# Second buffer for the sums of w2's pieces, a use-ordered list of their parts, and the fourth token sum split by VectorE in its PSUM bank

## The chip, the cores and the metric

The kernel runs on one core of a Trainium2 chip. The metric is the device time of one execution in microseconds, the median of several runs.

## The reference

Attention over 2 batches, 8 heads, 768 positions and head width 64, with a mask of 8 global and 96 local keys, feeds a mixture of four experts and then a gated block. What matters here is the expert part, computed for 1536 tokens with D = 512 and F = 1024, and the gated part behind it:

```python
for e in range(E):
    h = np.maximum(x @ w1[e], 0.0)
    out += p[:, e:e + 1] * (h @ w2[e])
...
a = x @ w1
b = x @ w2
h = a * b @ w3
return (h @ w_out).astype(np.float32)
```

## The kernel before, in words

**Precision and tiling.** Every fp32 operand is split into a high and a low part (`ah`, `al` for weights, `bh`, `bl` for tokens, `sh`, `sl` for hidden values). One product of two blocks is three matmuls of 128 x 128 by 128 x 384: high by high, low by high, high by low (lines 50 to 52). The high part is made by ScalarE, the low part by GpSimd or VectorE as "raw minus high".

**Seven products instead of eight.** The matrices are taken as 2 x 2 blocks, and a Strassen-Winograd scheme computes the four results c11, c12, c21, c22 from seven products. Weights enter as A11, A12, A22 and sums S1, S2, S3, S4; tokens as B11, B21, B22 and sums T1 to T4. Product 1 is A11 x B11, 2 is A12 x B21, 3 is S4 x B22, 4 is A22 x T4, 5 is S1 x T1, 6 is S2 x T2, 7 is S3 x T3. VectorE joins them: u2 from product 6, u3 from product 7, c22 from 5, c21 from 4, c12 from 3.

**Two halves.** The 1536 tokens are worked in two halves of 768. The first half of the dense part runs until about 477 us. The second half, t = 1, runs the four experts with `second_expert` and then `gated(1)`; the change touches only these.

**One second-half expert.** TensorE first works four groups i0 to i0+3 with w1 (seven products of two k-steps each; a group needs one set of split weights, loaded by SyncE with `load_split` from DRAM, in three ring slots). After each group ScalarE and VectorE rectify c11, c21, c22, which are B11, B21, B22 of the next matrix, and form the sums T1 to T4 of the rectified results (`rectified_sum`): T1 and T2 into `b_sum`, T3 and T4 into `raw[2]`. ScalarE takes the high part of each (`sum_high`), GpSimd the low part (`sum_low`). Then come two groups of w2, j and j+1, with seven products of four k-steps each, k being the group that the tokens come from (`down_group`).

**w2's pieces.** w2 comes in four pieces n0 to n0+3 per expert (two k-steps each), loaded raw into `raw[0]` and `raw[1]` in turn (`load_piece`), because `raw[2]` serves T3 and T4. GpSimd forms S1 to S4 of a piece in four operations (`down_sums`; S1, S2, S4 in `a_sum`, S3 in the piece itself). The piece is split in four parts, numbered by `PARTS`: 0 is A11, A12; 1 is S1, S2; 2 is A22, S3; 3 is S4. ScalarE makes the high part (`down_high`, line 1191), GpSimd the low part (`down_low`, line 1197), in order of piece and then of part. `a_sum` is one buffer, so the sums of a piece wait for the low parts of the one before.

**Order.** Every engine runs one queue written out by hand, in order, and they meet only through counting semaphores. `second_expert_gpsimd`, `second_expert_scalar`, `kept_sums` and `second_expert` are these queues for an expert. `snap` copies product 1 from its bank into `s1`, two buffers by parity of the group. Later `keep_h11` puts the rectified c11 there. `down_snap` does what `snap` does, for w2's groups. SyncE's queue is `sync`: a load whose wait is not met holds all loads behind it.

Of the kernel before, what the change touches and what calls it, by code (L numbers as in the profile page):

```python
# [28 lines left out]
E = 4  # L29
# [788 lines left out]
DOWN_ORDER = (1, 6, 2, 7, 5, 4, 3)  # L818
DOWN_SUMS = ("u2", "u3", "c22", "c21", "c12")
# [3 lines left out]
class Dense:  # L823
# [24 lines left out]
    def __init__(self, nc, sem, lay, bank, weights, folded, gates_dram, x_dram, x_stored, out, fold, g_stored):  # L848
# [55 lines left out]
        self.t_made, self.t_high, self.t_low = sem("t_made"), sem("t_high"), sem("t_low")  # L904
# [47 lines left out]
    def wait_split(self, eng, m):  # L952
        kind, n = self.pieces()[m]
        if kind == "up":
            eng.wait_ge(self.a_raw_low, n + 1)
        elif kind == "down":
            eng.wait_ge(self.dn_low, len(PARTS) * n + 3)
        else:
            eng.wait_ge(self.w2_low, self.w2_count(kind, n) + 1)
# [78 lines left out]
    def sync(self, sp):  # L1038
# [115 lines left out]

    def down_sums(self, pool, n):

        nc, c = self.nc, 4 * n
        raw, s = self.raw_of("down", n), self.a_sum
# [3 lines left out]
        if n:  # L1162
            pool.wait_ge(self.dn_low, len(PARTS) * n)
# [9 lines left out]
    def down_part(self, n, p):  # L1173
# [5 lines left out]
        return self.a_sum[:, to.start - S1 * QUART:to.stop - S1 * QUART], to  # L1179
# [13 lines left out]
    def down_low(self, pool, n, p):  # L1193
        src, to = self.down_part(n, p)
        s = self.slot_down(n)
        pool.wait_ge(self.dn_high, len(PARTS) * n + p + 1)
# [91 lines left out]
    def portion_t2(self, dve, k):  # L1288
        at = slice(k * TT, (k + 1) * TT)
        dve.wait_ge(self.b_summed, 12 + 4 * k + 1)  # L1290
        dve.wait_ge(self.t_low, 4 * KH * E)
# [53 lines left out]
    def bank_free(self, pe, i, c):  # L1345

        if i % UPS < 4 * E and i >= UPS:
            pe.wait_ge(self.t_made, self.t_count(i, {12: T1, 22: T2, 11: T3, 21: T4}[c]))
# [85 lines left out]

    def down_group(self, pe, j, p, ks=range(KH)):
# [12 lines left out]
        for k in ks:  # L1448
            i, n = UPS + KH * e + k, 2 * j + k // 2
            s = self.slot_down(n)  # L1450
            pe.wait_ge(self.dn_low, len(PARTS) * n + [a in part for part in PARTS].index(True) + 1)
            if b >= T1:
                pe.wait_ge(self.t_low, self.t_count(i, b))
# [8 lines left out]
    def second_expert(self, pe, e):  # L1462
# [82 lines left out]
    def gated(self, pe, t):  # L1545
# [77 lines left out]
    def snap(self, act, i):  # L1623
# [3 lines left out]
        elif i >= UPS + 2 and i < UPS + KH * E:  # L1627
            act.wait_ge(self.t_made, self.t_count(i - 2, T1))
# [50 lines left out]
    def t_raw(self, b):  # L1679
        return {T1: self.b_sum[:, 0:TT], T2: self.b_sum[:, TT:2 * TT], T3: self.raw[2][:, 0:TT],  # L1680
                T4: self.raw[2][:, TT:2 * TT]}[b]

    def sum_high(self, act, i, b):
        act.wait_ge(self.t_made, self.t_count(i, b))
        self.nc.scalar.activation(self.sh[b][i % KH][:, :], self.t_raw(b), ACT.Copy).then_inc(self.t_high, 1)  # L1685

    def down_snap(self, act, j):
        e, d = divmod(j, DOWNS)
        act.wait_ge(self.dn_product, self.dn_count(j, 1))
        act.wait_ge(self.t_made, self.t_count(UPS + KH * e + 2 + d, T1))  # L1690
        self.nc.scalar.activation(self.s1[d][:, :], self.bank[3 * d][:, 0:TT], ACT.Copy).then_inc(self.dn_snapped, 1)

    def second_expert_scalar(self, act, e):
        i0, n0 = UPS + KH * e, 4 * e
        for g in range(KH):
# [3 lines left out]
            if g:  # L1699
# [3 lines left out]
                if g >= 2:  # L1703
                    self.down_high(act, n0 + g - 2, 0)
# [17 lines left out]
        for n in (n0 + 2, n0 + 3):  # L1722
            for p in range(len(PARTS)):
                self.down_high(act, n, p)
        self.down_snap(act, DOWNS * e + 1)

    def second_gated_scalar(self, act):
# [151 lines left out]
    def sum_low(self, pool, i, b):  # L1879
        k = i % KH  # L1880
        pool.wait_ge(self.t_high, self.t_count(i, b))
        if b == T4 and k:
            for s in range(2):
                pool.wait_ge(self.y_stored[s], 16 * (ROWS_OUT // 2))
        self.nc.gpsimd.tensor_tensor(self.sl[b][k][:, :], self.t_raw(b), self.sh[b][k][:, :].bitcast(F32),  # L1885
                                     ALU.subtract).then_inc(self.t_low, 1)

    def sums_low(self, pool, i):
        for b in (T1, T2, T3, T4):
# [676 lines left out]
```

## Time and profile before

| | us |
|---|---|
| median of 3 runs (850.46 to 852.68) | 850.75 |
| the profiled execution, its own time | 854.38 |
| its span, first to last instruction | 852.8 |
| TensorE matmuls busy | 805.7 |
| GpSimd busy | 513.2 |
| VectorE busy | 451.9 |
| ScalarE busy | 334.1 |

The mean clock granted to TensorE was 0.981 of full speed. The engines overlap, so the busy times do not add up to the span. In the rows, PE is TensorE, DVE is VectorE, ACT is ScalarE, POOL is GpSimd and SP is SyncE; L1197 is line 1197 of the kernel. A row of a timeline gives the start, the duration, the engine, the line, the operation, output and inputs, and, in brackets, how long the engine idled before and what ended that.

### The profile page before, as it was taken

To read this page: it belongs to the slowest core of one execution; us is meant where nothing else is said; L and a number is where in the kernel's file an instruction comes from. 1 tells how busy PE (TensorE), PEld (TensorE's weight loads), DVE (VectorE), ACT (ScalarE), POOL (GpSimd) and SP (SyncE) were. 2 spreads that over 40 slices of the span, in tenths; PEclk is the share of its full clock that TensorE was granted. 3 is DMA by queue.
4 is the path that set the end of the run, shared out by engine and by line. 5 is a ranking of instruction groups with operands and counts; after the bars stand their busy time and mean duration, and the time that the engine had idled before them with its cause. 6 is when DMAs were issued, how large, how long until landed. Compare 5 with 4: busy or idle time off the path is not lost.

```text
span 852.8 us, 13816 instructions
## 1 busy us (share of the span) xinstructions
PE 805.7 (94%) x4702; PEld 756.8 (89%) x4702; DVE 451.9 (53%) x1002; ACT 334.1 (39%) x706; POOL 513.2 (60%) x476
## 2 busy tenths in 40 slices
PE   9999989999999999999999988996998898899997
PEld 7667758999999999998998988996997898888986
DVE  6776675514425425438664472475485375476620
ACT  4477873513314314323433362163063154322211
POOL 3478995784684675684965189189269449712200
PEclk9999999999999999999999998999999899899999
DMA  8924456773482473561996314634542552556501
GB/s 309 336 101 158 154 201 235 309 282 120 170 324 88 178 296 116 180 267 44 351 375 242 90 66 139 216 109 134 191 138 78 170 193 75 161 195 230 181 14 65
DMA packets 49563, 155.18 MB, mean 182 GB/s; under 512 B 5952, under 2 KB 7248, under 8 KB 49488
## 3 DMA queue, kind: packets, MB, share of 16 engines
q1 hardware_dynamic: 45104, 145.67, 47.5%
q10 hardware_dynamic: 4320, 8.52, 2.9%
q8 instruction: 43, 0.70, 0.3%
q0 software_dynamic: 64, 0.03, 0.1%
q14 instruction: 32, 0.26, 0.1%
HBM read 103.31 MB, written 50.88 MB: 181 GB/s over the span
## 4 chain that ended last, share of the span: by engine, by line
PE 69%; POOL 19%; DVE 5%; issue 3%; ACT 2%; DMA 1%; DVEq 0%; SPq 0%; ACTq 0%; POOLq 0%
PE bank L50 22%; PE bank L52 22%; PE bank L51 22%; POOL al L1197 6%; POOL sl L1885 5%; POOL pr L490 2%; PE bank L602 1%; PE bank L619 1%; PE bank L592 1%; POOL bl L1254 1%; POOL a_sum L1166 1%; POOL raw L1168 1%; POOL a_sum L1171 1%; POOL a_sum L1169 1%; DMA fold_mt_raw<-m3t 1%
## 5 line engine op out<-in xcount | busy, mean ns | idle before, releaser
L50 PE MATMUL bank<-bh,ah 128*128 128x384 f32 x672 | 226.3, 337 | 5.4 <-issue 1.8
L52 PE MATMUL bank<-bh,al 128*128 128x384 f32 x672 | 225.7, 336 | 0.0
L51 PE MATMUL bank<-bl,ah 128*128 128x384 f32 x672 | 225.5, 336 | 0.0
L50 PEld LDWEIGHTS bank<-bh,ah 128*128 128x128 f32 x672 | 126.8, 189 | 7.9 <-DVE hl L2227 2.4
L51 PEld LDWEIGHTS bank<-bl,ah 128*128 128x128 f32 x672 | 126.7, 189 | 0.1
L52 PEld LDWEIGHTS bank<-bh,al 128*128 128x128 f32 x672 | 126.6, 188 | 0.0
L1208 POOL TENSOR_TENSOR w2l<-raw,w2h 128x1024 fp32r<-128x1024 f32 x24 | 57.8, 2414 | 96.1 <-ACT w2h L1203 95.8
L50 PE MATMUL bank<-sh,ah 128*128 128x384 f32 x224 | 80.5, 359 | 26.1 <-POOL al L1197 22.8
L52 PE MATMUL bank<-hh,w2l 128*128 128x384 f32 x256 | 85.6, 335 | 0.0
L51 PE MATMUL bank<-hl,w2h 128*128 128x384 f32 x256 | 85.6, 335 | 0.0
L50 PE MATMUL bank<-hh,w2h 128*128 128x384 f32 x256 | 85.6, 334 | 0.0
L1150 POOL TENSOR_TENSOR al<-raw,ah 128x512 fp32r<-128x512 f32 x48 | 61.0, 1290 | 37.8 <-ACT ah L1130 37.5
L51 PE MATMUL bank<-sl,ah 128*128 128x384 f32 x224 | 79.2, 353 | 0.0
L52 PE MATMUL bank<-sh,al 128*128 128x384 f32 x224 | 78.9, 352 | 0.0
L1885 POOL TENSOR_TENSOR sl<-b_sum,sh 128x384 fp32r<-128x384 f32 x32 | 31.7, 1011 | 75.7 <-ACT sh L1685 75.7
L1634 ACT ACTIVATE parts<-bank 128x384 f32<-128x384 f32 x48 | 23.4, 488 | 124.2 <-PE bank L52 124.2
L50 PEld LDWEIGHTS bank<-sh,ah 128*128 128x128 f32 x224 | 45.2, 202 | 29.9 <-POOL al L1197 25.4
L490 POOL TENSOR_TENSOR pr<-pr,rden 128x512 f32<-128x512 f32 (+1 forms) x48 | 45.5, 972 | 9.0 <-DVE rden L558 9.0
L1998 DVE SCALAR_TENSOR_TENSOR hl<-bank,hh 128x384 fp32r<-128x384 f32 x64 | 35.3, 551 | 26.6 <-ACT hh L1643 26.2
L2019 DVE TENSOR_TENSOR bank<-bank,gate 128x384 f32<-128x384 f32 x24 | 13.4, 560 | 65.9 <-PE bank L52 65.9
L50 PEld LDWEIGHTS bank<-hh,w2h 128*128 128x128 f32 x256 | 48.1, 188 | 0.0
L51 PEld LDWEIGHTS bank<-hl,w2h 128*128 128x128 f32 x256 | 48.1, 188 | 0.0
(157 smaller groups left out, 1679.4 us busy)
## 6 DMA issues: line engine op xcount, KB each, us to landing
raw<-weights SPq DMA_DIRECT2D x56, 512.0 KB, 3.5
splits<-ah SPq DMA_DIRECT2D x24, 896.0 KB, 4.1
splits<-al SPq DMA_DIRECT2D x24, 896.0 KB, 6.4
ah<-splits SPq DMA_DIRECT2D x48, 256.0 KB, 3.4
al<-splits SPq DMA_DIRECT2D x48, 256.0 KB, 4.2
ah<-splits SPq DMA_DIRECT2D x24, 384.0 KB, 4.9
al<-splits SPq DMA_DIRECT2D x24, 384.0 KB, 6.2
k<-k SPq DMA_DIRECT2D x8, 704.0 KB, 6.5
```

Of the source, the lines that this page charges most:

```text
L50: nc.tensor.matmul(out, wh, xh, start=start, stop=False, skip_group_check=adds_on)
L51: nc.tensor.matmul(out, wh, xl, start=False, stop=False, skip_group_check=adds_on)
L52: return nc.tensor.matmul(out, wl, xh, start=False, stop=stop, skip_group_check=adds_on)
L490: self.nc.gpsimd.tensor_tensor(probs, probs, scale, ALU.mult).then_inc(self.normed, 1)
L592: last = self.nc.tensor.matmul(self.scores_of(u, h), self.q[s][head, i * P:(i + 1) * P], self.k[s][head, key0:key0 + self.width(u)], start ...
L1150: last = nc.gpsimd.tensor_tensor(self.al[s][:, c], self.raw_of("up", g)[:, c], self.ah[s][:, c].bitcast(F32), ALU.subtract)
L1197: self.nc.gpsimd.tensor_tensor(self.al[s][:, to], src, self.ah[s][:, to].bitcast(F32), ALU.subtract).then_inc(self.dn_low, 1)
L1208: self.nc.gpsimd.tensor_tensor(self.w2l[:, c], self.raw_of(kind, n)[:, :], self.w2h[:, c].bitcast(F32), ALU.subtract).then_inc(self.w2_low, 1)
L1634: self.nc.scalar.activation(self.s1[i % 2][:, :], self.bank[self.banks(i)[0]][:, 0:TT], ACT.Copy).then_inc(self.snapped, 1)
L1885: self.nc.gpsimd.tensor_tensor(self.sl[b][k][:, :], self.t_raw(b), self.sh[b][k][:, :].bitcast(F32), ALU.subtract).then_inc(self.t_low, 1)
L1998: self.nc.vector.scalar_tensor_tensor(self.hidden(self.hl, i, c), self.c_of(i, c), 0.0, self.hidden(self.hh, i, c).bitcast(F32), ALU.max, ...
L2019: nc.vector.tensor_tensor(bank, bank, gate, ALU.mult).then_inc(self.dn_scaled, 1)
```

## The change

- `down_sums` writes the sums of odd pieces to `raw[2]` and those of even pieces to `a_sum` (`sums_of`), so that a piece waits for the one two before it. GpSimd forms the sums of the next expert's first two pieces behind the current expert.
- The parts of an expert's four pieces are split in the order `DOWN_PARTS`, which runs over pairs of (piece, part), interleaved otherwise than before with the T sums in the queues of ScalarE and GpSimd.
- T3 goes to `s1[i % 2]`, and T4 is written over c21 in its PSUM bank. VectorE makes T4's low part (`t4_split_low`), and a semaphore of its own counts it. GpSimd is left with T1, T2, T3; in the last group T2 comes ahead of T1.
- `snap` and `down_snap` wait for GpSimd's low part of T3 of the group that had this `s1` before.
- TensorE's product orders change in w2's first group j and at the start of the second `gated`.
- SyncE asks for the splits of groups 4 and 5 of the last stage before the piece of w_out that stood between them.

```diff
+DOWN_PARTS = ((0, 0), (0, 2), (0, 1), (0, 3), (1, 0), (1, 1), (1, 2), (1, 3), (2, 0), (2, 1), (3, 0), (3, 1), (2, 2),
+              (3, 2), (2, 3), (3, 3))
...
-        self.load_splits(sp, i0 + 3)
+        for f in range(3, 6):
+            self.load_splits(sp, i0 + f)
         self.load_piece(sp, m + 2)
-        self.load_splits(sp, i0 + 4)
+        self.load_splits(sp, i0 + 6)
         self.load_piece(sp, m + 3)
-        for f in range(5, KF):
-            self.load_splits(sp, i0 + f)
+        self.load_splits(sp, i0 + 7)
...
+    def sums_of(self, n):
+        return self.raw[2][:, 0:3 * QUART] if n % 2 else self.a_sum[:, :]
...
-        if n:
-            pool.wait_ge(self.dn_low, len(PARTS) * n)
+        if n >= 2:
+            pool.wait_ge(self.dn_low, max(self.part_count(n - 2, 1), self.part_count(n - 2, 3)))
...
         self.down_group(pe, j, 5, (0, 1))
-        self.down_group(pe, j, 2, (0, 1))
+        self.down_group(pe, j, 2, (0, 1, 2))
         self.down_group(pe, j, 6, (3,))
-        self.down_group(pe, j, 2, (2, 3))
+        self.down_group(pe, j, 2, (3,))
+        self.down_group(pe, j, 5, (2,))
         self.down_group(pe, j, 7)
-        self.down_group(pe, j, 5, (2, 3))
+        self.down_group(pe, j, 5, (3,))
         self.down_group(pe, j, 4)
...
+            self.product1(pe, i0 + 1)
             self.product5(pe, i0, (0,))
             self.product6(pe, i0, (0,))
             self.product2(pe, i0)
-            self.product1(pe, i0 + 1)
             self.product2(pe, i0 + 1)
             self.product5(pe, i0, (1,))
             self.product6(pe, i0, (1,))
-            self.product5(pe, i0 + 1)
+            self.product5(pe, i0 + 1, (0,))
             self.product7(pe, i0)
-            self.product6(pe, i0 + 1)
+            self.product5(pe, i0 + 1, (1,))
             self.product4(pe, i0)
             self.product3(pe, i0)
+            self.product6(pe, i0 + 1)
...
         elif i >= UPS + 2 and i < UPS + KH * E:
-            act.wait_ge(self.t_made, self.t_count(i - 2, T1))
+            act.wait_ge(self.t_low, self.low_count(i - 2, T3))
...
-    def t_raw(self, b):
-        return {T1: self.b_sum[:, 0:TT], T2: self.b_sum[:, TT:2 * TT], T3: self.raw[2][:, 0:TT],
-                T4: self.raw[2][:, TT:2 * TT]}[b]
+    def t_raw(self, i, b):
+        return {T1: self.b_sum[:, 0:TT], T2: self.b_sum[:, TT:2 * TT], T3: self.s1[i % 2][:, :], T4: self.c_of(i, 21)}[b]
...
-            act.wait_ge(self.t_made, self.t_count(UPS + KH * e + 2 + d, T1))
+            act.wait_ge(self.t_low, self.low_count(UPS + KH * e + 2 + d, T3))
...
+        order = DOWN_PARTS[0:2], DOWN_PARTS[2:4], DOWN_PARTS[4:5], DOWN_PARTS[5:8]
...
-                    self.down_high(act, n0 + g - 2, 0)
+                    for m, p in order[2 * g - 4]:
+                        self.down_high(act, n0 + m, p)
...
-                for p in range(1, len(PARTS)):
-                    self.down_high(act, n0 + g - 2, p)
+                for m, p in order[2 * g - 3]:
+                    self.down_high(act, n0 + m, p)
...
-                self.out_high(act, "last", 4 + f - 2 - f // 4)
+                self.out_high(act, "last", 2 + f - f // 4)
...
     def second_expert_gpsimd(self, pool, e):
...
+        self.sums_low(pool, i0, T1, T2, T3)
+        self.parts_low(pool, e, 0, 2)
+        self.sums_low(pool, i0 + 1, T1, T2, T3)
+        self.parts_low(pool, e, 2, 5)
+        self.sums_low(pool, i0 + 2, T1, T2)
+        self.parts_low(pool, e, 5, 6)
+        self.down_sums(pool, n0 + 2)
+        self.sums_low(pool, i0 + 2, T3)
+        self.parts_low(pool, e, 6, 7)
+        self.sums_low(pool, i0 + 3, T2, T1, T3)
+        self.parts_low(pool, e, 7, 11)
+        self.down_sums(pool, n0 + 3)
+        self.parts_low(pool, e, 11, 16)
         if e < E - 1:
             self.down_sums(pool, n0 + 4)
+            self.down_sums(pool, n0 + 5)
...
+    def t4_split_low(self, dve, i):
+        k = i % KH
+        dve.wait_ge(self.t_high, self.t_count(i, T4))
...
+        self.nc.vector.tensor_tensor(self.sl[T4][k][:, :], self.t_raw(i, T4), self.sh[T4][k][:, :].bitcast(F32),
+                                     ALU.subtract).then_inc(self.t4_low, 1)
...
         self.add_u3_c22(dve, i)
+        if i % KH:
+            self.t4_split_low(dve, i - 1)
         self.add_c21(dve, i)
```

## Rows read from the trace of the kernel before

**Rows 1.** The page, busy time and share of the span of each engine
```profile
PE 805.7 (94%) x4702; PEld 756.8 (89%) x4702; DVE 451.9 (53%) x1002; ACT 334.1 (39%) x706; POOL 513.2 (60%) x476
```

**Rows 2.** TensorE's waits from 480 to 853 us: total us, times, longest
```profile
PE bank L50 <- POOL al L1197: 22.8, 8, 3.6
PE bank L50 <- POOL sl L1885: 3.2, 3, 1.1
```

**Rows 3.** TensorE's timeline of the last second-half expert
```profile
707.51 0.33 PE L50 MATMUL bank<-sh,ah 128*128 128x384 f32 x1
...
712.54 0.34 PE L52 MATMUL bank<-sh,al 128*128 128x384 f32 x1
715.13 0.44 PE L50 MATMUL bank<-sh,ah 128*128 128x384 f32 x1 [2.26 <-POOL al L1197]
...
719.08 0.42 PE L50 MATMUL bank<-sh,ah 128*128 128x384 f32 x1 [1.05 <-POOL sl L1885]
...
732.78 0.69 PE L50 MATMUL bank<-sh,ah 128*128 128x384 f32 x1 [3.55 <-POOL al L1197]
733.27 0.52 PE L51 MATMUL bank<-sl,ah 128*128 128x384 f32 x1
...
748.88 0.34 PE L50 MATMUL bank<-bh,ah 128*128 128x384 f32 x1
```

**Rows 4.** GpSimd's timeline from 487 to 753 us
```profile
487.24 1.99 POOL L1885 TENSOR_TENSOR sl<-b_sum,sh 128x384 fp32r<-128x384 f32 x2 [16.82 <-ACT sh L1685]
...
554.73 1.99 POOL L1885 TENSOR_TENSOR sl<-b_sum,sh 128x384 fp32r<-128x384 f32 x2 [19.25 <-ACT sh L1685]
...
622.31 2.00 POOL L1885 TENSOR_TENSOR sl<-b_sum,sh 128x384 fp32r<-128x384 f32 x2 [19.31 <-ACT sh L1685]
...
690.84 2.00 POOL L1885 TENSOR_TENSOR sl<-b_sum,sh 128x384 fp32r<-128x384 f32 x2 [20.30 <-ACT sh L1685]
...
697.30 1.29 POOL L1197 TENSOR_TENSOR al<-raw,ah 128x512 fp32r<-128x512 f32 x1 [2.21 <-ACT ah L1191]
698.56 1.99 POOL L1885 TENSOR_TENSOR sl<-b_sum,sh 128x384 fp32r<-128x384 f32 x2
...
715.03 1.28 POOL L1197 TENSOR_TENSOR al<-raw,ah 128x512 fp32r<-128x512 f32 x1
716.28 0.73 POOL L1197 TENSOR_TENSOR al<-a_sum,ah 128x256 fp32r<-128x256 f32 x1
...
720.83 0.73 POOL L1166 TENSOR_TENSOR a_sum<-raw 128x256 f32<-128x256 f32 x1
...
723.84 1.31 POOL L1197 TENSOR_TENSOR al<-raw,ah 128x512 fp32r<-128x512 f32 x1
...
752.38 1.41 POOL L1279 TENSOR_TENSOR bl<-x,bh 128x384 fp32r<-128x384 f32 x1 [1.18 <-ACT bh L1274]
```

**Rows 5.** ScalarE's timeline, the fourth group's snap and the first of w2
```profile
701.96 0.47 ACT L1634 ACTIVATE parts<-bank 128x384 f32<-128x384 f32 x1
...
712.57 0.50 ACT L1691 ACTIVATE parts<-bank 128x384 f32<-128x384 f32 x1
```

**Rows 6.** VectorE's timeline, u3 of the fourth group and a split from SBUF
```profile
707.71 0.56 DVE L1964 TENSOR_TENSOR parts<-bank,parts 128x384 f32<-128x384 f32 x1
...
752.92 1.27 DVE L1279 TENSOR_TENSOR bl<-b_sum,bh 128x384 fp32r<-128x384 f32 x1
```

**Rows 7.** SyncE's issues in the last stage; DMA issues from 550 to 760 us (last row)
```profile
774.15 0.32 SPq L968 DMA_DIRECT2D raw<-folded  x1
774.51 0.43 SPq L1030 DMA_DIRECT2D ah<-splits  x1
...
raw<-weights SPq DMA_DIRECT2D x10, 512.0 KB, 3.5
```

**Rows 8.** TensorE's timeline of the last stage, two of its four waits
```profile
762.87 0.44 PE L50 MATMUL bank<-bh,ah 128*128 128x384 f32 x1 [1.39 <-DVE hl L2227]
...
781.12 0.41 PE L50 MATMUL bank<-bh,ah 128*128 128x384 f32 x1 [1.83 <-issue]
```

More of the change, by code:

```diff
@@ L956, in wait_split @@
         elif kind == "down":
-            eng.wait_ge(self.dn_low, len(PARTS) * n + 3)
+            eng.wait_ge(self.dn_low, self.part_count(n, 2))
         else:
@@ L1153, in up_half_low, with part_count @@
             last.then_inc(self.a_raw_low, 1)
+    @staticmethod
+    def part_count(n, p):
+        e, j = divmod(n, 2 * DOWNS)
+        return len(DOWN_PARTS) * e + DOWN_PARTS.index((j, p)) + 1
+    def sums_of(self, n):
+        return self.raw[2][:, 0:3 * QUART] if n % 2 else self.a_sum[:, :]
     def down_sums(self, pool, n):
         nc, c = self.nc, 4 * n
-        raw, s = self.raw_of("down", n), self.a_sum
+        raw, s = self.raw_of("down", n), self.sums_of(n)
         a11, a12, a22, a21 = [raw[:, q * QUART:(q + 1) * QUART] for q in range(4)]
@@ L1433, in t_count, with low_count @@
         return 4 * (self.h_count(i) - KH * E) + b - T1 + 1
+    def low_count(self, i, b):
+        order = (T2, T1, T3) if i % KH == KH - 1 else (T1, T2, T3)
+        return 3 * (self.h_count(i) - KH * E) + order.index(b) + 1
     def down_group(self, pe, j, p, ks=range(KH)):
@@ L1450, in down_group @@
             s = self.slot_down(n)
-            pe.wait_ge(self.dn_low, len(PARTS) * n + [a in part for part in PARTS].index(True) + 1)
-            if b >= T1:
-                pe.wait_ge(self.t_low, self.t_count(i, b))
+            pe.wait_ge(self.dn_low, self.part_count(n, [a in part for part in PARTS].index(True)))
+            if b == T4:
+                pe.wait_ge(self.t4_low, KH * e + k + 1)
+            elif b >= T1:
+                pe.wait_ge(self.t_low, self.low_count(i, b))
             else:
@@ L1721, in second_expert_scalar @@
             self.sum_high(act, i, b)
-        for n in (n0 + 2, n0 + 3):
-            for p in range(len(PARTS)):
-                self.down_high(act, n, p)
+        for m, p in DOWN_PARTS[8:]:
+            self.down_high(act, n0 + m, p)
         self.down_snap(act, DOWNS * e + 1)
@@ L1881, in sum_low, with sums_low, parts_low @@
         pool.wait_ge(self.t_high, self.t_count(i, b))
[L1882 to L1885, printed above, removed]
+        self.nc.gpsimd.tensor_tensor(self.sl[b][k][:, :], self.t_raw(i, b), self.sh[b][k][:, :].bitcast(F32),
                                      ALU.subtract).then_inc(self.t_low, 1)
[L1888 to L1889 removed]
+    def sums_low(self, pool, i, *bs):
+        for b in bs:
             self.sum_low(pool, i, b)
+    def parts_low(self, pool, e, first, last):
+        for m, p in DOWN_PARTS[first:last]:
+            self.down_low(pool, 4 * e + m, p)
     def second_expert_gpsimd(self, pool, e):
         i0, n0 = UPS + KH * e, 4 * e
[L1894 to L1908 removed]
+        self.sums_low(pool, i0, T1, T2, T3)
[11 more added lines that the diff above has]
+        self.parts_low(pool, e, 11, 16)
         if e < E - 1:
             self.down_sums(pool, n0 + 4)
+            self.down_sums(pool, n0 + 5)
     def gpsimd(self, pool):
@@ L1924, in gpsimd @@
             self.b_split_low(pool, on, b, 2)
-        self.down_sums(pool, 0)
+        for n in range(2):
+            self.down_sums(pool, n)
         for e in range(E):
@@ L2032, in rectified_sum @@
         c = {T1: 12, T2: 22, T3: 11, T4: 21}[b]
-        less = {T1: self.s1[i % 2][:, :], T2: self.t_raw(T1), T3: self.t_raw(T2), T4: self.t_raw(T2)}[b]
+        less = self.s1[i % 2][:, :] if b == T1 else self.t_raw(i, min(b - 1, T2))
         q = self.t_count(i, b)
@@ L2039, in rectified_sum @@
             dve.wait_ge(self.t_made, self.t_count(i, min(b - 1, T2)))
-        if q > 4:
-            dve.wait_ge(self.t_low, q - 4)
+        if b == T4:
+            dve.wait_ge(self.h_low[21], self.h_count(i) + 1)
+        elif b <= T2 and q > 4:
+            dve.wait_ge(self.t_low, self.low_count(i - 1, b))
             dve.wait_ge(self.t_made, self.t_count(i - 1, T4))
@@ L2123, in second_expert_vector @@
         self.kept_sums(dve, i, False)
+        self.t4_split_low(dve, i)
         for j in (DOWNS * e, DOWNS * e + 1):
```

41 lines of the change are left out of this document (16 added, 25 removed).

## The prediction

> **What bounds the kernel now.** I read the page's busy shares first: TensorE is busy for 94% of the span [rows 1], so only its idle time and its slow time can be won. The table of waits from 480 us on names the releasers: 22.8 us in 8 waits on `al` from GpSimd's line 1197 and 3.2 us in 3 waits on `sl` from its line 1885, 26.0 us in all [rows 2]. TensorE's timeline of the last second-half expert shows where: at 715.13 (2.26 us idle), at 719.08 (1.05) and at 732.78 (3.55), then matmuls of 0.69 and 0.52 us where 0.33 is usual [rows 3]. That is the lower clock level, 1.2 instead of 2.4 GHz, right after the idle time. A stall is thus paid twice.
>
> The full pace is (712.54 - 707.51)/29 = 0.1734 us a matmul [rows 3]. A product (6 matmuls, 2 k-steps) takes 1.04 us, a product of four k-steps 2.08. An expert has 28 of the former and 7 of the latter, 336 matmuls, 58.3 us. In the last expert the second matrix starts at 707.51 after 26 products (27.05 us), so the expert began at 680.46; the next stage begins at 748.88: 68.4 us [rows 3]. The other three follow from the first `sl` of each, 487.24, 554.73, 622.31, 690.84: 67.5, 67.6 and 68.5 us [rows 4]. The sum is 272.0 us, the floor 4 x 58.3 = 233.1. So 38.9 us are lost: 26.0 idle, the rest the slower clock and the restarts.
>
> GpSimd is behind because of its own queue. Its costs end to end, from starts: a 384-wide low part 0.98, a 512-wide one 1.25, a 256-wide one 0.69, the four sums of a piece 723.84 - 720.83 = 3.0 us [rows 4]. Per expert: 16 x 0.98 + 12 x 1.25 + 4 x 0.69 + 4 x 3.0 = 45.5 us, nearly all of it between 697.30 and 736, while it idles 20 us before 690.84.
>
> **The change, step by step.** I walk the last expert with the same durations.
>
> *GpSimd.* Four of the 16 `sl` go to VectorE, -3.9 us per expert. Of the four sets of sums one ran behind the previous expert, in the 20 us of idle time; now two do, 3.0 us more out of the queue: the second `S` buffer (`raw[2]`) allows it, because T3 and T4 leave it. For expert 0 the idle time before 487.24 takes the extra set. The new queue from 697.30: part (0,0), (0,2) to 699.8; T1, T2, T3 of group 1 to 702.8 (before: its T4 ended at 702.5); (0,1), (0,3) to 704.7; (1,0), whose high part ScalarE gives near 705.0, to 706.3; T1, T2 of group 2 to 708.3; (1,1), whose high part follows T4's near 708.8, to 710.2; sums of piece 2 to 713.2; T3 to 714.2; (1,2) to 715.4; then group 3's T2 from 715.6 (its high part waits in ScalarE's queue, below) to 716.6, T1, T3 to 718.5; (1,3), (2,0), (2,1), (3,0) to 723.0; sums of piece 3 to 726.0; (3,1) to 728.0; the rest to 732.
>
> *VectorE.* `t4_split_low` costs 0.56, the same as the other bank readers [rows 6], in each group, just ahead of `add_c21`. There VectorE idles 0.86 us in every group for TensorE; the low part fits with 0.4 us left, so it costs nothing in groups 0 and 1.
>
> *ScalarE.* `snap(i+2)` now waits for GpSimd's T3 of group i, because T3 lives in `s1`. In group 3 that moves the snap from 701.96 [rows 5] to 702.8. Behind it, `kept_high(22)`, VectorE's `kept_low(22)`, c12 and all sums move by 0.7 us, and u3 of group 3 goes from 707.71 [rows 6] to 708.2. Product 4 needs it at 708.55 and gets it at 708.8: **0.25 us** of stall. `down_snap` moves from 712.57 [rows 5] to 714.2, after T3 of group 2; product 2 wants it at 714.5 and gets it at 714.75: **0.23**.
>
> *TensorE's order for piece group j.* Product 6's k=2 needs (1,1) at 712.7 and has it since 710.2: the stall of 2.26 is gone. Product 6's k=3 needs T2 of group 3; T2 now goes first and k=2 of product 2 stands in front, so it is wanted at 716.3 and there at 716.65: **0.35**. Product 4 waits for u3, made from product 7, and has only half a product of cover now where it had a whole one: 0.56 + two handovers against 0.52, **0.3**. Product 3 of j ends at 725.3. For group j+1, (3,0) is wanted at 726.3 and ready at 723.0, which removes the 3.55 us; (3,1) is wanted at 728.4 and ready at 728.0; the rest has 2 us or more. So j+1 runs through, and the expert ends at 725.3 + 14.6 = 739.9 instead of 748.9: 59.4 us, of which 1.1 are stalls. All four are short; the matmuls behind the waits of 1.05 and 1.39 us took 0.42 and 0.44, not 0.69 [rows 3, 8], so I charge no slow clock. The gain is 272.0 - 4 x 59.4 = **34.4 us**.
>
> *Loads.* Piece 3's load waits for (1,2) at 715.4; at 3.5 us a piece [rows 7] it lands at 719, ahead of ScalarE's need at 720 to 721. Pieces 4 and 5 are asked for at 729 and 731 and land by 735, and GpSimd's two sets of sums behind them end near 741, while its next expert's work begins at 750.
>
> *The last stage.* TensorE sits at 781.12 for 1.83 us, released by nothing on an engine [rows 8]. The SyncE rows show what: `load_piece` holds the queue until 774.15, and the splits for group 4 are issued only behind it, from 774.5 [rows 7], though their slot was free near 769. The new order puts groups 4 and 5 ahead. It removes the issue gap of 2.0 us and 10 matmuls at 0.32 instead of 0.17, 1.5 us, and restarts of 0.2: 3.7 us. The piece then is asked for near 778 and wanted by ScalarE at 791. The other product orders: the wait for `snap` at 753.9 stays, since that snap stands in ScalarE's queue behind portions of x; product 7 and product 4 wait 0.4 us each for u2 and u3, and the 1.39 at 762.87 [rows 8] shrinks to 0.4. Net 0.2. Together **3.9 us**. The rewritten number of `out_high` gives the same four values as before.
>
> **The sum.** 34.4 + 3.9 = 38.3 us off the profiled execution: span 852.8 - 38.3 = 814.5, its own time 854.4 - 38.3 = 816.1. That execution lies 3.6 us over the median of the runs, so the median goes 850.75 - 38.3 = 812.4. I say 812.5.
>
> **Bounds of what the trace does not show.** VectorE splits T4 straight from its bank after having written it there. Nearest rows: 0.56 for a bank reader; above, a low part with both inputs in SBUF that took 1.27 us beside a GpSimd one of 1.41 [rows 4, 6]. Below there is nothing: no row of this width is under 0.55. I take 0.56, since this operation reads its bank too. The upper end is 0.7 us more each, 0.3 beyond the slack, and is rival 3. For the four small stalls the ends are nothing (4.5 us less) and the whole of what each replaces, the old waits, which is a rival.
>
> The case shown by those rows bears on a rule. The Trainium skill, page SBUF — State Buffer, section "Who interferes with whom", says that a VectorE instruction with two SBUF inputs and a GpSimd one that reads SBUF block each other for the whole instruction, and one with a single SBUF input does not. The rows of 1.27 and 1.41 agree. By that page the moved split, with one input in a bank, never collides.
>
> **Rivals.**
> 1. *A remainder of the GpSimd wait.* Margins are thin: 0.4 us for (3,1), and T2 of group 3 is late already. If each handover takes 0.1 to 0.2 us more, one wait of 2 us comes back, and with it some 10 matmuls at the lower clock, 1.5 us. Per expert 3.5, in all 14: 826. For it: only thin margins; against: GpSimd reaches (1,1) 4.9 us and (3,0) 9.7 us earlier. Half of that, 819, is likelier. Together 0.20.
> 2. *All covered.* The small stalls fall into slack that I overrate by a few tenths: 812.4 - 4.5 = 808. Chance 0.10.
> 3. *The split of T4 is held up by GpSimd after all.* It then takes up to 1.27 us instead of 0.56 [rows 6], with 0.4 of slack, and c21 comes 0.3 to 0.4 late in three groups: 1.2 an expert, 5 us, 817. The page named above speaks against it. Chance 0.05.
> 4. *Slower.* One mechanism: the new ring, GpSimd's T3, `snap(i+2)`, product 2, sums, and T3 again. It decides when T3 of group i ends later than TensorE's need for the snap, now 702.8 against 705.6, and it is worse than before only when it costs over 9.6 us an expert, each of two snaps 4.8, so T3 at 710. At 12 us an expert: 850.75 + 4 x 2.4 - 3.9 = 856. Nothing in the rows makes GpSimd 7 us late before the middle of the expert. Chance 0.02.
> 5. *The change does nothing:* the waits are GpSimd's and its queue is shortened, so only if a load took their place exactly. Chance 0.01.
>
> The forecast itself holds 0.62, with 809 to 816. For 8 in 10 I take 808 to 824, which reaches through rival 3 and half of rival 1. Under 0.3%, 2.6 us, a measurement of this kernel can't tell from no change. Faster 0.97, same 0.01, slower 0.02.
>
> **What would show it.** TensorE's waits on `al` gone from 26.0 to near nothing; from one expert's first `sl` to the next 59 to 60 us; its granted clock 1.00 throughout these stages; GpSimd idle under 12 us between experts; `down_snap` released by GpSimd; no wait near the fourth group of the last stage. A wait over 1 us on `al` in group j+1, or a snap that stands for GpSimd for over 2 us, makes the forecast wrong.

## The result and the profile after

The changed kernel takes **817.6 us** (median of 4 runs, 817.35 to 817.82), the kernel before beside it on the same chip 851.2 us (4 runs, 850.46 to 852.68). The ratio is 0.960, 95% interval 0.959 to 0.962. The forecast was 812.5 with 808 to 824. The profiled execution has a time of 817.35 us and a span of 815.8 us at a mean granted clock of 0.998; before it was 854.38 us, 852.8 us and 0.981.

The page of the changed kernel, answering to [rows 1]:

```profile
span 815.8 us, 13801 instructions
PE 794.8 (97%) x4702; PEld 744.4 (91%) x4702; DVE 461.9 (57%) x1018; ACT 331.9 (41%) x706; POOL 500.3 (61%) x460
```

Sixteen instructions went from GpSimd to VectorE, and TensorE is busy for 97% of the span. What it still waits for, from 460 us to the end, answering to [rows 2] (columns: total us, times, longest):

```profile
PE bank L50 <- ACT parts L1660: 1.2, 1, 1.2
PE bank L50 <- DVE parts L2128: 0.7, 1, 0.7
PE bank L50 <- POOL sl L1908: 0.7, 4, 0.2
PE bank L50 <- DVE hl L2265: 0.3, 1, 0.3
PE bank L50 <- DVE parts L1975: 0.2, 1, 0.2
```

The 22.8 us on `al` are gone, and 0.7 of the 3.2 us on `sl` is left. GpSimd's timeline gives the pace of the experts by the first `sl` of each, and the fourth group, the sums of piece 3 and the work behind the last expert, answering to [rows 4]:

```profile
485.66 1.99 POOL L1908 TENSOR_TENSOR sl<-b_sum,sh 128x384 fp32r<-128x384 f32 x2 [13.78 <-ACT sh L1710]
...
545.42 1.99 POOL L1908 TENSOR_TENSOR sl<-b_sum,sh 128x384 fp32r<-128x384 f32 x2 [11.50 <-ACT sh L1710]
...
605.15 2.00 POOL L1908 TENSOR_TENSOR sl<-b_sum,sh 128x384 fp32r<-128x384 f32 x2 [10.57 <-ACT sh L1710]
...
664.93 2.00 POOL L1908 TENSOR_TENSOR sl<-b_sum,sh 128x384 fp32r<-128x384 f32 x2 [11.40 <-ACT sh L1710]
...
689.78 1.99 POOL L1908 TENSOR_TENSOR sl<-b_sum,sh 128x384 fp32r<-128x384 f32 x2 [0.24 <-ACT sh L1710]
...
697.12 0.75 POOL L1180 TENSOR_TENSOR raw<-raw 128x256 f32<-128x256 f32 x1
...
706.82 4.54 POOL L1293 TENSOR_TENSOR bl<-x,bh 128x384 fp32r<-128x384 f32 x4
```

From expert to expert it is 59.76, 59.73 and 59.78 us, where the forecast had 59.4. GpSimd idles 10.6 to 13.8 us ahead of each, no longer 16.8 to 20.3.

TensorE's timeline of the last second-half expert and the start of the last stage, answering to [rows 3] and the first row of [rows 8]:

```profile
690.94 0.41 PE L50 MATMUL bank<-sh,ah 128*128 128x384 f32 x1 [0.17 <-POOL sl L1908]
...
695.03 0.34 PE L52 MATMUL bank<-sh,al 128*128 128x384 f32 x1
695.50 0.45 PE L50 MATMUL bank<-sh,ah 128*128 128x384 f32 x1
...
711.02 0.45 PE L50 MATMUL bank<-sh,ah 128*128 128x384 f32 x1 [0.66 <-DVE parts L2128]
...
715.29 0.33 PE L50 MATMUL bank<-bh,ah 128*128 128x384 f32 x1
...
720.86 0.44 PE L50 MATMUL bank<-bh,ah 128*128 128x384 f32 x1 [1.25 <-ACT parts L1660]
...
729.60 0.44 PE L50 MATMUL bank<-bh,ah 128*128 128x384 f32 x1 [0.34 <-DVE hl L2265]
```

A stall can stand as two starts that lie apart: a matmul follows the one before it after 0.17 us, and from 695.03 to 695.50 it is 0.47, so 0.30 us were lost although the row has no bracket. That is the stall ahead of product 4. The three waits of 1.05 to 3.55 us of [rows 3] have become four of 0.17 to 0.30. New is 0.66 us at 711.02. The last stage begins at 715.29; in the profile before it was 748.88.

ScalarE's two snaps, answering to [rows 5], now stand for GpSimd's T3 (the `sl` of L1908) as forecast:

```profile
676.96 0.49 ACT L1660 ACTIVATE parts<-bank 128x384 f32<-128x384 f32 x1 [1.37 <-POOL sl L1908]
...
688.39 0.49 ACT L1716 ACTIVATE parts<-bank 128x384 f32<-128x384 f32 x1 [2.72 <-POOL sl L1908]
```

TensorE's granted clock, in the table of stretches (columns: stretch, its length, busy time and count of PE, PEld, DVE, ACT and POOL, clock, DMA share, GB/s), for the first 60 us and for the experts:

```profile
0.00:60.00 60.00, 54.90 (x322) 41.92 (x322) 44.27 (x134) 32.93 (x79) 33.50 (x38) 1.00 0.73 265
...
475.00:715.00 240.00, 237.79 (x1345) 232.35 (x1345) 162.47 (x306) 102.81 (x226) 165.90 (x173) 1.00 0.46 155
```

**Where the time came from, by the two profiled executions.** They are 854.38 - 817.35 = 37.0 us apart. The four experts went from 272.0 to 240.0 us (three of 59.8 and a last one of 60.7): 32.0. The last stage went from 852.8 - 748.9 = 103.9 to 815.8 - 715.3 = 100.5 us: 3.4. The other 1.6 us lie ahead of the experts, in stages that the change does not touch: the profile before had this row for its first 60 us, with 312 matmuls at a clock of 0.97, where the changed kernel has 322 at 1.00. It is no property of the kernel before: two of the experiments below on the changed kernel, `set_in_queue` and `old_loads`, have the same 0.97 there in their profiled executions, and the experts begin 1.6 to 1.8 us later in them.

```profile
0.00:60.00 60.00, 54.86 (x312) 41.90 (x313) 43.71 (x134) 32.14 (x77) 32.20 (x37) 0.97 0.71 255
```

### The profile page after: what moved, and what is told of

The parts are those of the page before. It is cut to its first block and busy times, and to the rows that moved or that the text cites. A ratio compares the mean times of both kernels' runs of the same rounds, so it can differ in the third digit from the quotient of the medians.

```text
span 815.8 us, 13801 instructions
## 1 busy us (share of the span) xinstructions
PE 794.8 (97%) x4702; PEld 744.4 (91%) x4702; DVE 461.9 (57%) x1018; ACT 331.9 (41%) x706; POOL 500.3 (61%) x460
## 5 line engine op out<-in xcount | busy, mean ns | idle before, releaser
L50 PE MATMUL bank<-sh,ah 128*128 128x384 f32 x224 | 76.2, 340 | 2.1 <-DVE parts L2128 0.7
L52 PE MATMUL bank<-sh,al 128*128 128x384 f32 x224 | 75.0, 335 | 0.0
L51 PE MATMUL bank<-sl,ah 128*128 128x384 f32 x224 | 75.0, 335 | 0.0
L1211 POOL TENSOR_TENSOR al<-raw,ah 128x512 fp32r<-128x512 f32 (+1 forms) x48 | 57.3, 1209 | 19.8 <-ACT ah L1205 19.8
L1908 POOL TENSOR_TENSOR sl<-b_sum,sh 128x384 fp32r<-128x384 f32 x32 | 31.9, 1018 | 48.2 <-ACT sh L1710 48.2
L52 PEld LDWEIGHTS bank<-hh,w2l 128*128 128x128 f32 x256 | 48.0, 188 | 0.0
```

The costliest lines, as they stand in the source:

```text
L50: nc.tensor.matmul(out, wh, xh, start=start, stop=False, skip_group_check=adds_on)
L51: nc.tensor.matmul(out, wh, xl, start=False, stop=False, skip_group_check=adds_on)
L52: return nc.tensor.matmul(out, wl, xh, start=False, stop=stop, skip_group_check=adds_on)
L1211: self.nc.gpsimd.tensor_tensor(self.al[s][:, to], src, self.ah[s][:, to].bitcast(F32), ALU.subtract).then_inc(self.dn_low, 1)
```

## The experiments

Each ran beside the kernel before on one chip (its medians there 851.2, 851.5 and 851.6 us). First two edits that carry one part of the change onto the kernel before, then edits that take one part out of the changed kernel, then attempts at the stalls that are left.

**One part alone, on the kernel before.** The split of T4 by VectorE from its bank, and nothing else:

```diff
-        for b in (T1, T2, T3, T4):
+        for b in (T1, T2, T3):
             self.sum_low(pool, i, b)
...
         self.add_u3_c22(dve, i)
+        if i % KH:
+            self.t4_split_low(dve, i - 1)
         self.add_c21(dve, i)
```

> The kernel before with one part of the change: T4 is written over c21 in its bank and split by VectorE; T3 stays in raw[2], one buffer of sums, all old orders. Queue theory (TensorE waits as long as GpSimd's queue is late): GpSimd's queue loses 0.98 us per T4, but all four sets of sums stay where they were. From the rows of before, (1,1) is split by 713.1 against a need at 712.7 (0.4 us of stall), T1 and T2 of group 3 by 717.0 against 715.8 (1.2), (3,0) by 729.7 against 727 (2.8), and some 1.5 us of slow clock: 6 us lost per expert where the kernel before loses 9.7. So about 4 us an expert, 16 in all: 835, with waits on al and sl of about 17 us. Rival (T4's move carries it, the second buffer is not needed): waits under 3 us and a time near 822, which is this change without its loads.

Measured 838.1 us (836.9 to 839.6), ratio 0.984 with 0.979 to 0.989: 13 us faster than before, where 16 were expected. TensorE's waits from 460 us on:

```profile
PE bank L50 <- POOL al L1197: 12.2, 8, 2.7
PE bank L50 <- POOL sl L1890: 4.3, 4, 1.1
```

Four instructions fewer for GpSimd in an expert, 3.9 us, took the waits on `al` from 22.8 to 12.2 us, but all eight remain. So the shift of work gives over a third of the gain and does not carry the change.

The new order of SyncE's loads alone:

```diff
-        self.load_splits(sp, i0 + 3)
+        for f in range(3, 6):
+            self.load_splits(sp, i0 + f)
         self.load_piece(sp, m + 2)
-        self.load_splits(sp, i0 + 4)
+        self.load_splits(sp, i0 + 6)
         self.load_piece(sp, m + 3)
-        for f in range(5, KF):
-            self.load_splits(sp, i0 + f)
+        self.load_splits(sp, i0 + 7)
```

> The kernel before with SyncE's new order in the last stage alone. If the piece of w_out held up the splits of group 4: the wait of 1.83 us and ten slow matmuls near it go, 3.7 us, 847.5, and TensorE's waits on al stay at 26 us. Rival (the splits land late because the DMA queues are full, wherever they are issued): the wait stays or moves to the next group, and the time is 851.

Measured 848.2 us (846.0 to 851.0), ratio 0.997 with 0.995 to 0.999, so 3 us faster, near the 847.5 expected; the issue wait is gone and GpSimd's waits stay (23.3 us on `al`). So the rival of full DMA queues falls. The opposite edit, the old order in the changed kernel:

> The changed kernel with SyncE's old order of loads in the last stage, the same part as in loads_alone but without that kernel's scatter. If the load queue's order costs what my prediction took from the rows, 3.7 us, this runs in 821.3 and TensorE waits some 1.8 us ahead of group 4 of the last stage for nothing on an engine, with about ten matmuls at the lower clock behind it. Rival (the expert part now runs ahead by 32 us and the loads have room): 817.6.

Measured 820.7 us (819.6 to 821.6), 3.1 us slower than the change. Its TensorE timeline has the old stall, and SyncE's shows its cause, a piece's load that holds the splits of group 4 until 743.02; in the changed kernel they are issued from 735.10 on.

```profile
749.83 0.41 PE L50 MATMUL bank<-bh,ah 128*128 128x384 f32 x1 [2.02 <-issue]
```

```profile
742.66 0.32 SPq L970 DMA_DIRECT2D raw<-folded  x1
743.02 0.43 SPq L1032 DMA_DIRECT2D ah<-splits  x1
```

The medians of both signs of the edit say 3 us, where the forecast had 3.7, but the traces split that otherwise. In `old_loads` the last stage took 102.8 us on the trace, in the changed kernel 100.5: 2.3 us. The rest of the distance lies ahead of the experts, in the 1.8 us of its profiled execution named above; of its four executions two took 819.6 and 820.0 us at a mean clock of 0.999, two 821.5 and 821.6 at 0.996 and 0.997. In the kernel before, the stage took 103.9 us with the old order and 100.5 with the new one: 3.5 us. The difference is the clock behind the wait. After 1.83 us of waiting it fell in the profile of the kernel before (first row), after 2.02 us it did not in `old_loads` (second row), so the ten slow matmuls expected there did not come:

```profile
784.00:789.00 5.00, 5.00 (x25) 5.00 (x24) 3.63 (x7) 0.98 (x2) 0.00 (x0) 0.81 1.00 372
```

```profile
754.00:759.00 5.00, 5.00 (x31) 5.00 (x30) 3.13 (x6) 0.93 (x2) 0.00 (x0) 1.00 1.04 404
```

**The second set of sums back in the queue.** The second `S` buffer stays, but the sums of piece 1 are formed inside the expert instead of behind the previous one:

```diff
         self.parts_low(pool, e, 2, 5)
+        self.down_sums(pool, n0 + 1)
         self.sums_low(pool, i0 + 2, T1, T2)
...
             self.down_sums(pool, n0 + 4)
-            self.down_sums(pool, n0 + 5)
...
-        for n in range(2):
-            self.down_sums(pool, n)
+        self.down_sums(pool, 0)
```

> The changed kernel with one thing undone: the sums of each expert's second piece are formed inside the expert, ahead of group 2's T1 as before, and not behind the expert before. Queue theory: 3.0 us more in GpSimd's queue between (1,0) and T1 of group 2. T3 of group 2 then ends near 717.2 in the times of my forecast, where down_snap needs it at 714.3: product 2 of j stalls some 3 us longer, with up to 1.5 us of slow clock behind it. 3 to 4.5 us an expert, 12 to 18 in all: 830 to 836. Rival (most of the gain is T4's): under 1 us an expert, 818 to 821.

Measured 829.7 us (828.2 to 831.0), ratio 0.974 with 0.970 to 0.979: 12.1 us slower than the change, at the lower end of the 12 to 18 us expected and far from the rival. TensorE's waits, and the row of `down_snap` in the last expert:

```profile
PE bank L50 <- ACT parts L1716: 9.9, 4, 2.5
```

```profile
700.76 0.49 ACT L1716 ACTIVATE parts<-bank 128x384 f32<-128x384 f32 x1 [4.55 <-POOL sl L1908]
```

`down_snap` stands 4.55 us for GpSimd's T3 (2.72 in the changed kernel) and TensorE 2.5 us for `down_snap` in each expert. This is the ring of rival 4, started on purpose: 3.0 us of delay in GpSimd's queue cost 10.9 us in four experts by the trace (250.9 us against 240.0), 2.7 us each; 1.6 of the profiled execution's distance lies ahead of the experts, where the edit does nothing. The ring is real but needs a delay that the change does not have.

What the order of parts in `DOWN_PARTS` is worth by itself, no run shows: the second `S` buffer, the move of T3 and T4 out of `raw[2]` and the new order were only taken together, apart from the pieces tried here.

**The reordered parts, one at a time.** T1 ahead of T2 again in an expert's last group:

```diff
-        order = (T2, T1, T3) if i % KH == KH - 1 else (T1, T2, T3)
+        order = (T1, T2, T3)
...
-        self.sums_low(pool, i0 + 3, T2, T1, T3)
+        self.sums_low(pool, i0 + 3, T1, T2, T3)
```

> The changed kernel with T1 ahead of T2 in the last group of each expert. Queue theory: T2 of group 3 already comes 0.2 to 0.3 us late (TensorE's wait on sl), so 0.98 us more is paid in full: 4 x 1.0, 821.5, and four waits on sl of about 1.2 us. Rival (the wait of 0.2 us is a handover and not lateness; there is slack elsewhere): 817.6.

Measured 820.5 us (820.4 to 822.2), ratio 0.964: 2.9 us slower, where 3.9 were expected. Its four waits on `sl` sum to 3.4 us instead of 0.7, which is nearly all of it; the longest is 0.9 us.

The old product order within group j:

```diff
-        self.down_group(pe, j, 2, (0, 1, 2))
+        self.down_group(pe, j, 2, (0, 1))
         self.down_group(pe, j, 6, (3,))
-        self.down_group(pe, j, 2, (3,))
-        self.down_group(pe, j, 5, (2,))
+        self.down_group(pe, j, 2, (2, 3))
         self.down_group(pe, j, 7)
-        self.down_group(pe, j, 5, (3,))
+        self.down_group(pe, j, 5, (2, 3))
```

> The changed kernel with the old order of TensorE's products in w2's group j. Product 6's last step then wants T2 of group 3 half a microsecond earlier, and pays that: +0.5 us; product 4 has a whole product of cover for u3 again: -0.3. Queue theory: +0.2 us an expert, 818.4, with the wait on sl at 0.7 us each and no gap ahead of product 4. Rival (the new order was needed to cover the wait on T2): +0.5 and more an expert and no gain at product 4, 820 to 822.

Measured 818.2 us (818.0 to 819.3): 0.6 us slower than the change, as expected, with two ranges that nearly touch. The gap ahead of product 4 closes, and the waits on `sl` grow to 2.7 us: what one end of the order gives, the other takes.

The old product order at the start of the last stage:

```diff
-            self.product1(pe, i0 + 1)
             self.product5(pe, i0, (0,))
             self.product6(pe, i0, (0,))
             self.product2(pe, i0)
+            self.product1(pe, i0 + 1)
...
-            self.product5(pe, i0 + 1, (0,))
+            self.product5(pe, i0 + 1)
             self.product7(pe, i0)
-            self.product5(pe, i0 + 1, (1,))
+            self.product6(pe, i0 + 1)
             self.product4(pe, i0)
             self.product3(pe, i0)
-            self.product6(pe, i0 + 1)
```

> The changed kernel with the old order of products at the start of the last stage. By my walk the new one saves 0.2 us: 817.8, the same within what can be measured; the wait at the head of group 2 grows from 0.34 back to 1.4 us and the two gaps of 0.3 us before products 7 and 4 close. Rival (the new order is worth the whole 1.05 us by which that wait shrank): 818.7.

Measured 818.1 us (818.0 to 818.4): 0.5 us slower, between the 0.2 expected and the rival's 1.05. The wait for `hl` is 1.4 us again instead of 0.3, and the wait for the snap 0.8 instead of 1.2.

**The stalls that are left.** If GpSimd's T3 makes the snaps late, bringing it forward must close the gaps ahead of product 4 of group 3, product 2, and T2's product together:

```diff
-        self.parts_low(pool, e, 0, 2)
+        self.parts_low(pool, e, 0, 1)
         self.sums_low(pool, i0 + 1, T1, T2, T3)
-        self.parts_low(pool, e, 2, 5)
-        self.sums_low(pool, i0 + 2, T1, T2)
+        self.parts_low(pool, e, 1, 5)
+        self.sums_low(pool, i0 + 2, T1, T2, T3)
         self.parts_low(pool, e, 5, 6)
         self.down_sums(pool, n0 + 2)
-        self.sums_low(pool, i0 + 2, T3)
```

> The changed kernel with GpSimd's low part of T3 moved up in its queue: in group 1 ahead of part (0,2), in group 2 ahead of part (1,1) and the sums of piece 2. If the ring (T3, snap, product 2) costs what my walk says, the gaps of 0.2 us before product 4 of group 3 and before product 2 of j close, and T2's high part is no longer held up behind down_snap, so its wait on sl goes too: 0.2 + 0.25 + 0.3 us an expert, 3 us in all, 814.6. Rival (the gaps are not the ring's): 817.6, with the gaps still there; or slower, where (1,1), now 1 us later, is needed sooner than I think: up to 4 x 0.6, 820.

Measured **813.2 us** (812.9 to 813.4), ratio 0.956 with 0.953 to 0.957: 4.4 us faster than the change, where 3.0 were expected. ScalarE's row of `down_snap` in the last expert, and TensorE's ahead of product 4:

```profile
683.03 0.49 ACT L1716 ACTIVATE parts<-bank 128x384 f32<-128x384 f32 x1 [0.60 <-PE bank L52]
```

```profile
690.98 0.34 PE L52 MATMUL bank<-sh,al 128*128 128x384 f32 x1
691.44 0.45 PE L50 MATMUL bank<-sh,ah 128*128 128x384 f32 x1
```

`down_snap` now waits for its own product, no longer for GpSimd, and the waits on `sl` are gone. Only the gap of 0.46 - 0.17 = 0.29 us ahead of product 4 remains in each expert, and in the last one a wait of 0.52 us for u3.

The half of it for group 1 alone, T3 of group 2 left where the change has it:

```diff
-        self.parts_low(pool, e, 0, 2)
+        self.parts_low(pool, e, 0, 1)
         self.sums_low(pool, i0 + 1, T1, T2, T3)
-        self.parts_low(pool, e, 2, 5)
+        self.parts_low(pool, e, 1, 5)
```

> Only the first half of the former: T3 of group 1 ahead of part (0,2). Snap of the fourth group should start 0.9 us earlier after its product 1, and only the gap before product 4 of group 3 should close: 0.2 us an expert, 816.8. Rival (the delay comes from VectorE's queue with one operation more and not from the snap): the gap stays, 817.6.

Measured 816.4 us (816.1 to 817.2): 1.2 us faster than the change, with only the first of the gaps closed. The rest of the 4.4 us belongs to T3 of group 2.

With `t3_early` and one k-step of the next group's product 1 in front of product 4, as cover for u3:

```diff
         self.down_group(pe, j, 5, (3,))
+        self.down_group(pe, j + 1, 1, (0,))
         self.down_group(pe, j, 4)
         self.down_group(pe, j, 3)
-        for p in DOWN_ORDER:
+        self.down_group(pe, j + 1, 1, (1, 2, 3))
+        for p in DOWN_ORDER[1:]:
             self.down_group(pe, j + 1, p)
```

> T3 moved up as in t3_early, and in each expert the first step (k=0) of product 1 of group j+1 put ahead of product 4 of group j. The gap of 0.29 us before product 4 is VectorE making u3 out of product 7 (0.56 us and two handovers) behind half a product of cover; with a whole one it should close: 4 x 0.29 us below t3_early, 812.0. Rival (the gap is the switch to another bank and not cover): 813.2, with the gap in its place.

Measured **812.1 us** (811.9 to 812.9), 1.1 us less, as expected, but not as four gaps of 0.29. By the traces the first three experts took 58.24 us instead of 58.67, so that each gave 0.43, and the last one nothing (59.45 after 59.47): its gap closed, and its wait for u3 near the end grew from 0.52 to 0.94 us.

```profile
705.59 0.44 PE L50 MATMUL bank<-sh,ah 128*128 128x384 f32 x1 [0.94 <-DVE parts L2129]
```

**The end of the last expert.** It takes 60.7 us in the changed kernel and the others 59.8, in `t3_early` 59.5 and 58.7. VectorE's timeline of `t3_early` has the sums that it forms there for the next stage, while GpSimd splits B11 to T1 without a pause:

```profile
700.57 1.15 DVE L1299 TENSOR_TENSOR x<-x 128x384 f32<-128x384 f32 x1
...
703.72 1.28 DVE L1312 TENSOR_TENSOR x<-b_sum,x 128x384 f32<-128x384 f32 x1
704.92 1.38 DVE L1317 TENSOR_TENSOR x<-x,b_sum 128x384 f32<-128x384 f32 x1
```

So GpSimd was held back: on top of `t3_early`, in the last expert it waits for VectorE's sums ahead of the rest of its splits.

```diff
+        if e == E - 1:
+            self.parts_low(pool, e, 11, 14)
+            self.portion_low(pool, self.nc.gpsimd, B11, 0)
+            self.parts_low(pool, e, 14, 16)
+            self.portion_low(pool, self.nc.gpsimd, B21, 0)
+            pool.wait_ge(self.b_summed, 16)
...
-        for b in (B11, B21, B22, T1):
+        for b in (B22, T1):
```

> T3 moved up as in t3_early, and in the last expert alone GpSimd splits B11 and B21 of the next stage's tokens earlier and then stands still until VectorE has made T3 and T4 of them. VectorE's five operations with both inputs in SBUF took 0.98 to 1.38 us there instead of 0.55 beside a busy GpSimd. Contention theory: with GpSimd idle, the operations that make T3 and T4 (1.28 and 1.38 us in t3_early) drop to 0.55 to 0.8 us, and TensorE's wait of 0.52 us for u3 near the end of the last expert goes: 812.7. Rival (the wait comes from VectorE's order of work, not from its durations): the wait stays near 0.5 us, 813.2.

Measured 815.6 us (813.2 to 816.3), where 812.7 was expected: a miss, slower than `t3_early`. VectorE's rows show both halves of it, and TensorE's the price:

```profile
703.65 0.73 DVE L1312 TENSOR_TENSOR x<-b_sum,x 128x384 f32<-128x384 f32 x1
705.29 0.56 DVE L1317 TENSOR_TENSOR x<-x,b_sum 128x384 f32<-128x384 f32 x1 [0.91 <-POOL bl L1293]
...
707.07 1.26 DVE L1293 TENSOR_TENSOR bl<-b_sum,bh 128x384 fp32r<-128x384 f32 x1
708.25 1.37 DVE L1293 TENSOR_TENSOR bl<-x,bh 128x384 fp32r<-128x384 f32 x1
```

```profile
717.12 0.44 PE L50 MATMUL bank<-bh,ah 128*128 128x384 f32 x1 [1.81 <-ACT parts L1660]
```

The two sums fell from 1.28 and 1.38 to 0.73 and 0.56 us, and the wait for u3 went: the last expert took 58.8 us, the others 58.7. But GpSimd, let go later, now met both of VectorE's splits, 1.26 and 1.37 us (0.55 and 1.37 in `t3_early`). The snap came later, TensorE waited 1.81 instead of 1.2 us for it, and behind that wait the granted clock was 0.66 in this kernel (19 matmuls in 5 us) and 1.00 in `t3_early` (26), by the table of stretches of each:

```profile
717.00:722.00 5.00, 4.88 (x19) 4.69 (x20) 2.36 (x5) 0.59 (x2) 0.00 (x0) 0.66 0.10 37
```

```profile
717.00:722.00 5.00, 4.76 (x26) 4.11 (x25) 2.75 (x6) 0.53 (x1) 0.00 (x0) 1.00 0.20 77
```

Both edits together:

> Both of the former on top of t3_early. If the two gaps are separate, the gains add: 813.2 - 1.2 - 0.5 = 811.5. Rival (one hides the other): 812.0.

Measured 811.5 us (810.8 to 812.7), ratio 0.954 with 0.952 to 0.956. The intervals overlap with `t3_early_cover` (812.1), so by the times the hold is not shown to help or to harm there. The traces do show what it does to the last expert, 58.7 us instead of 59.5, with the snap's wait at 1.2 us; the gain of the profiled execution is lost again ahead of the experts, which begin 1.0 us later in it. Both versions beat both kernels: the best is 6.1 us under the change and 40.1 under the kernel before that ran beside it.

## Why the forecast was right, and 5 us low

**The bound: right.** In the experts TensorE lost time for GpSimd's queue alone. All waits on `al` went, and the expert's time with them.

**The walk of GpSimd's queue: right to 0.2 us.** At the last expert the profile after runs 25.9 us ahead of the time axis on which the forecast was walked, that of the profile before. With that taken off, the snap of group 3 was expected at 702.8 - 25.9 = 676.9 and began at 676.96; `down_snap` at 688.3 and 688.39; T2 of group 3 at 689.7 and 689.78; the sums of piece 3 at 697.1 and 697.12; (3,1) ended at 702.3, expected 702.1. Starts read from one timeline, added end to end, carry a whole queue.

One of the forecast's own signs of being wrong did appear: a snap that stands for GpSimd for over 2 us. `down_snap` stood 2.72 us. The sign was badly chosen, for the same walk had put this snap at its place to 0.1 us. It measures how long ScalarE idled, and TensorE lost only 0.25 us by it.

**VectorE's split of T4 at 0.56 us: right, rival 3 fell.** The rows of tile `sl` on VectorE, by shape, with the shortest, the median and the longest in ns:

```profile
L2084 DVE TENSOR_TENSOR sl<-bank,sh x16: 545/547/558, 489.1 to 690.5; 128x384 fp32r<-128x384 f32 x16
```

None of the 16 came near 1.27 us. GpSimd worked beside 12 of them, and idled during the other four, the first of each expert. The measured 817.6 us lies at the 817 that rival 3 would give, but its mechanism is not there. By the Trainium skill, page SBUF — State Buffer, section "Who interferes with whom", a VectorE instruction with at most one SBUF input does not contend with GpSimd, outside the two-port modes; the trace agrees, with 558 ns as the longest.

**The small stalls: their places right, their sum low.** The forecast had 0.25, 0.23, 0.35 and 0.3, 1.1 us an expert. Read by starts they were 0.18 to 0.20 ahead of product 4 of group 3, 0.24 to 0.25 ahead of product 2, 0.15 to 0.18 idle for T2's product and 0.29 to 0.30 ahead of product 4. Behind each of them the next matmul also follows late, after 0.24 to 0.29 us instead of 0.17, about 0.1 us more, with a bracket or without. The forecast charged nothing for that. So an expert of 58.3 took 59.76 on the trace, 1.45 of loss, and the four experts 1.4 us more than forecast. The experiment that brings T3 forward gave 4.4 us for the part of these losses that hang on GpSimd, and the cover 1.1 for the last: 5.5 for a sum that the walk had put at 4.5.

**The last expert: missed.** It took 60.7 us, about 1 more than the others, 0.66 of it waiting for `parts` from VectorE (row 711.02). VectorE's last two sums for the next stage took 1.28 and 1.36 us beside GpSimd, where each took 0.55 in the profile before. Counted from the expert's start, VectorE now comes to these sums 8.6 us earlier and GpSimd to its splits of `bl` 3.4 us earlier, so that they run together. Before the change the last expert was no longer than the third (68.4 and 68.5 us), so there the cost was covered. The forecast never asked what GpSimd, once early, would do to VectorE at the end. `tail_hold` shows the mechanism: the rows fell to 0.73 and 0.56 us, and of the 0.8 us by which the last expert of `t3_early` exceeded the others 0.7 went. That the same holds for the whole 1 us of the changed kernel is argued from there.

**The last stage: 3.4 instead of 3.9.** The loads gave 3.1 instead of 3.7 by the medians of `old_loads`, and 2.3 of it in the stage itself. The forecast had put 1.5 us of slow matmuls behind the wait, which stood in the profile before and not in that of `old_loads`. The wait for the snap that the forecast kept as it was grew to 1.25 us, and the wait for `hl` fell from 1.39 to 0.34; `old_gated_order` prices the new product order at 0.5 where 0.2 was charged.

**The steps that failed.** The forecast lies 5.1 us under the measured median, and three terms make up nearly all of it. First, the gain of 272.0 - 4 x 59.4 = 34.4 us was mis-sized: on the profiled executions the experts gave 32.0, 2.4 less, of which the small stalls are 1.4 and the last expert 1.0. Second, the last stage gave 3.4 for 3.9, 0.5 less. Third, and this step failed in kind, is "That execution lies 3.6 us over the median of the runs, so the median goes 850.75 - 38.3". A gain worked out on an execution that was slow by itself was taken off a median that was not. The experts and the last stage together gained 32.0 + 3.4 = 35.4 us on the profiled executions, the medians 851.2 - 817.6 = 33.6: 1.8 us less. With the 0.4 by which the kernel before ran over 850.75 beside the change, 2.4 + 0.5 + 1.8 + 0.4 = 5.1.

Where such an excess sits can be read from `loads_alone`, whose trace is a second profile of the experts of the kernel before, since its edit begins behind them. It comes from an execution of 848.06 us, beside that kernel's median of 848.24. TensorE idled 6.9 us in the last expert in both profiles, on the same waits, yet the expert took 68.41 us in the profile before and 66.01 in the other. In the tables of stretches the granted clock is 0.95 and 1.00:

```profile
680.47:748.88 68.41, 61.55 (x338) 60.62 (x337) 41.68 (x80) 29.28 (x63) 47.63 (x50) 0.95 0.43 145
```

```profile
680.03:746.04 66.01, 59.12 (x338) 58.19 (x338) 43.05 (x80) 29.29 (x63) 47.97 (x50) 1.00 0.45 150
```

In all, the experts took 272.0 us in the one and 270.6 in the other, so 1.5 of the 1.8 us appear as a difference between two executions of the same code. Both are single executions, and the slow clock behind the issue wait of the last stage, some 1.2 us, is a draw of the same kind; how the 1.8 us divide exactly stays open. The end point did better than the difference: 816.1 us was worked out for the profiled execution and 817.35 measured, but this was partly luck: 1.6 us of that agreement came from the start, where the execution before had been slow.

## What to carry to other kernels

Walk the late engine's queue with its own starts and name what is late next: it placed every wait inside an expert to a few tenths. Where the profiled execution lies over the median, part of the loss read from it is that execution's own, so a change that removes the waits gains less on the median than on the profile. When an engine is freed, look at the end of the stage for what it will now run beside.

## What the runs showed of the hardware

The time of a kernel scatters with its waits, though not with them alone. The kernel before had runs from 848.0 to 854.6 us, with a mean granted clock from 0.990 down to 0.981; the changed kernel, with no wait over 1.25 us from 460 us on, from 817.35 to 817.82 at 0.998 to 0.999. `tail_hold`, with one wait of 1.81 us, ran from 813.2 us (0.998) to 816.3 (0.995). Behind the same waits, one expert ran at a granted clock of 0.95 in one execution and 1.00 in another, 2.4 us apart. A long wait costs a lower clock in some executions and not in others, so its price in one profile is one draw. The first 60 us show such a difference too, without any change of code there: 0.97 in three of the profiled executions, where the experts begin at 476.8 to 477.0 us, and 1.00 in that of the changed kernel, where they begin at 475.3.

VectorE's additions of 128x384 with both inputs in SBUF took 0.55 to 0.56 us with GpSimd at rest and up to 1.38 beside it, while the operation with one input in a bank stayed at 0.545 to 0.558 in all 16 cases, 12 of them beside a working GpSimd. Holding GpSimd back only moved such a collision onto the next pair of instructions.
